# Attention scores in bursts of three doubles, as 64-row matmuls in two halves of the array, over six PSUM banks

## What is computed

```python
scores = (1 / S) * np.matmul(z, z.transpose(0, 2, 1))      # z: (8, 3072, 64)
attn = np.maximum(scores, 0.0) ** 2
x = (u * np.matmul(attn, v)).reshape(B * S, D)             # u, v: (8, 3072, 256)

expert_idx = np.argmax(x @ w_gate, axis=1)                 # 8 experts
for i in range(N):                                         # rows in order, up to capacity each
    if counts[e] < capacity: disp[e, counts[e]] = x[i]; ...
h = np.maximum(np.einsum('ecd,edf->ecf', disp, w1), 0.0)   # w1: (8, 256, 1024)
y = np.einsum('ecf,efd->ecd', h, w2)
out[i] = gate_w[i] * y[expert_idx[i], pos[i]]              # rows that were kept, the rest 0
```

## Time and profile before

| | |
|---|---|
| median of three runs | 867.1 us |
| span of the profiled execution | 865.3 us |
| TensorE matmul busy | 853.5 us |
| TensorE weight load busy | 683.9 us |
| VectorE busy | 632.4 us |
| ScalarE busy | 574.7 us |
| GpSimd busy | 123.2 us |
| attention, until about | 609 us |

### The profile page before, as it was taken

How to read it: one execution, slowest core, us unless ns; L and a number is a source line. 1 busy time by engine, 2 the same in 40 slices (tenths; PEclk the granted TensorE clock), 3 DMA queues, 4 the chain that set the end, 5 groups by cost and what they waited for, 6 DMA issues and landing times.

```text
span 865.3 us, 22736 instructions
## 1 busy us (share of the span) xinstructions
PE 853.5 (99%) x7258; PEld 683.9 (79%) x7259; DVE 632.4 (73%) x1380; ACT 574.7 (66%) x874; POOL 123.2 (14%) x121
## 2 busy tenths in 40 slices
PE   6999999999999999999999999999999999999997
PEld 5888888888888888888888888888777777777776
DVE  7976777988889878887888798687464655565531
ACT  7978786868778779777778777678434434435422
POOL 1001102101101110110110110110112121211212
PEclk9999999999999999999999999999999999999999
DMA  7922343343312633312313313731625325415101
GB/s 274 372 70 94 87 129 136 100 135 117 118 46 97 240 108 97 115 49 92 115 50 98 107 53 108 264 82 40 145 65 171 102 80 158 142 46 152 55 18 36
DMA packets 104277, 98.62 MB, mean 114 GB/s; under 512 B 67149, under 2 KB 91802, under 8 KB 103232
## 3 DMA queue, kind: packets, MB, share of 16 engines
q1 hardware_dynamic: 99360, 85.71, 32.1%
q0 software_dynamic: 4896, 12.64, 4.0%
HBM read 40.03 MB, written 44.93 MB: 98 GB/s over the span
## 4 chain that ended last, share of the span: by engine, by line
PE 97%; DVE 2%; issue 1%; POOL 0%; ACT 0%; POOLq 0%; DVEq 0%; ACTq 0%
PE O L676 17%; PE O L678 17%; PE O L680 17%; PE Sc L786 14%; PE Sc L640 8%; PE Sc L641 8%; PE O L809 3%; PE O L813 3%; PE O L811 3%; PE M L809 2%; PE M L813 2%; PE M L811 2%; PE M L717 1%; PE M L615 0%; DVE zQ L904 0%
## 5 line engine op out<-in xcount | busy, mean ns | idle before, releaser
L676 PE MATMUL O<-vS,attn_hi 128*128 128x256 f16 x1332 | 363.0, 273 | 0.3 <-DVE vS L930 0.3
L680 PE MATMUL O<-vS,attn_lo 128*128 128x256 f16 x1332 | 363.0, 273 | 0.0
L678 PE MATMUL O<-vS,attn_hi 128*128 128x256 f16 x1332 | 363.0, 273 | 0.0
L462 ACT ACTIVATE Sc<-Sc 128x768 f32<-128x768 f32 x224 | 178.0, 795 | 86.3 <-PE Sc L641 78.4
L947 DVE TENSOR_TENSOR attn_lo<-attn,attn_hi 128x768 f16<-128x768 f32 x223 | 213.7, 958 | 7.7
L466 ACT ACTIVATE attn<-Sc 128x768 f32<-128x768 f32 x224 | 181.7, 811 | 7.1
L676 PEld LDWEIGHTS O<-vS,attn_hi 128*128 128x128 f16 x1332 | 130.2, 98 | 27.2 <-issue 0.4
L678 PEld LDWEIGHTS O<-vS,attn_hi 128*128 128x128 f16 x1332 | 130.3, 98 | 26.6
L640 PE MATMUL Sc<-zP 128*128 (+1 forms) x450 | 146.4, 326 | 2.1 <-DVE zP L911 1.3
L641 PE MATMUL Sc<-zQ,zP 128*128 (+1 forms) x450 | 146.4, 326 | 0.0
L941 DVE CAST attn_hi<-attn 128x768 f16<-128x768 f32 x223 | 123.7, 555 | 27.4 <-ACT attn L466 26.0
(11 more groups left out here) (155 smaller groups left out, 912.4 us busy)
## 6 DMA issues: line engine op xcount, KB each, us to landing
out<-empty SPq DMA_DIRECT2D x16, 1536.0 KB, 6.3
wraw<-in_moe_w SPq DMA_DIRECT2D x16, 1024.0 KB, 7.0
rawv<-in_v SPq DMA_DIRECT2D x14, 768.0 KB, 8.5
ubuf<-in_u SPq DMA_DIRECT2D x19, 384.0 KB, 3.1
disp<-vS SPq DMA_DIRECT2D x8, 774.0 KB, 9.1
rawz<-in_z SPq DMA_DIRECT2D x3, 768.0 KB, 6.0
xT<-xrow SPq DMA_TRANSPOSE x54, 2.4
disp<-xrow,slot POOLq DMA_INDIRECT x54, 2.8
```

Source lines behind the costliest of these rows:

```text
L462: act.activation(pair, pair, ACT.Relu).then_inc(s["relu_done"], 1)
L676: nc.tensor.matmul(o_part(t), hi, v[:, 0:D], start=c == 0 and j == 0 and t % 2 == 0, stop=False, skip_group_check=True)
L678: nc.tensor.matmul(o_part(t), hi, v[:, D:2 * D], start=False, stop=False, skip_group_check=True)
L680: ins = nc.tensor.matmul(o_part(t), lo, v[:, 0:D], start=False, stop=c == PAIRS - 1 and j == 1, skip_group_check=True)
```

## The change

Scores are computed as 64-row matmuls. For each double, each of its two key tiles has one half of the array (rows 0 to 63 for the first, 64 to 127 for the second) and a bank of its own, and gets three terms: high keys x high queries, high x low, low x high. The term low x low is gone. Each term is issued for both halves in turn. Three doubles are issued in one burst, at c = 0, 3, 6 and 9 (double c + 3 and the two after it), into six banks, so that PSUM has no banks left for `M`: logits, counts and norm sums lie in the first score bank, and the waits for that are new. Value matmuls keep their 128 rows.

Relu writes from PSUM to `attn`, square works there in place; the score banks wait for relu only. ScalarE's and VectorE's programs are reordered to the bursts, and VectorE's cast waits for the values of four doubles back (`weighed`). The queries of a group are copied by SyncE's DMAs into fixed buffers (`q_now` for the group, `q_next` and `k_next` for the first burst of the next one, which is issued at the end of the group before). The end of the loop is tested after double 6 instead of 5. `identh` is gone; `before` serves in its place. Some small tiles share memory now.

```diff
-LEAD = 3
+BURST = 3
+COUNTS_FROM = 48
+RING = 4
...
-        zsq = sb("zsq", [P, S // 2], BF16)
+        q_now = [sb(f"q_now{k}", [P, GROUP], F16) for k in range(2)]
+        q_next = [sb(f"q_next{k}", [P, GROUP], F16) for k in range(2)]
+        k_next = [sb(f"k_next{k}", [P, SLICE * P], F16) for k in range(2)]
...
-        identh = sb("identh", [P, P], F16)
...
-        Sp = ps("Sc", [P, 4, 512], F32)
-        Mp = ps("M", [P, 2, 512], F32)
+        Sp = ps("Sc", [P, 2 * BURST, 512], F32)
+
+        def half(r):
+            return slice(64 * r, 64 * r + 64)
+
+        def score_banks(c):
+            return slice(2 * (c % BURST), 2 * (c % BURST) + 2)
...
+        small_logits = Sp[:, 0, 0:TILES * 2 * E]
+        small_counts = Sp[:, 0, COUNTS_FROM:COUNTS_FROM + (TILES + 1) * E]
+        norm_sums = Sp[:, 0, 0:GROUP]
...
+            def queries(to, m, loaded):
+
+                for q, z16 in zip(to, (zP, zQ)):
+                    sp.dma_start(q[:, :], z16[:, bass.ds((m & 15) * GROUP, GROUP)]).then_inc(s[loaded], 16)
+
+            def first_keys(m):
+
+                for k, z16 in zip(k_next, (zP, zQ)):
+                    sp.dma_start(k[:, :], z16[:, bass.ds((m & 8) * (S // 8), SLICE * P)]
+                                 ).then_inc(s["loaded_k_next"], 16)
+
             def body(n, end):
                 g = n & 7
-                if not isinstance(n, int):
-
+                if isinstance(n, int):
+                    for key in ("khi_ready", "klo_ready"):
+                        sp.wait_ge(s[key], 2)
+                    first_keys(0)
+                else:
+
+                    wait_apart(sp, s["scores_ready"], n * PAIRS)
+                    queries(q_now, n, "loaded_q_now")
+                    wait_apart(sp, s["scores_ready"], n * PAIRS + BURST)
+                    for key in ("khi_ready", "klo_ready"):
+                        wait_apart(sp, s[key], ((n + 1) & 126) + 2)
+                    queries(q_next, n + 1, "loaded_q_next")
+                    only_if(sp, g == 7, lambda: first_keys(n + 1))
                     for t in range(TILES):
...
             def do_relu(K, c):
                 act.wait_ge(s["scores_ready"], K + 1)
-                pair = Sp[:, 2 * (c % 2):2 * (c % 2) + 2, 0:GROUP]
-                act.activation(pair, pair, ACT.Relu).then_inc(s["relu_done"], 1)
+                if not isinstance(K, int) or K >= BUFS:
+                    wait_apart(act, s["lo_done"], K - BUFS + 1)
+                act.activation(attn[:, c % BUFS, :, :], Sp[:, score_banks(c), 0:GROUP], ACT.Relu
+                               ).then_inc(s["relu_done"], 1)
 
             def do_square(K, c):
                 act.wait_ge(s["relu_done"], K + 1)
-                act.activation(attn[:, c % BUFS, :, :], Sp[:, 2 * (c % 2):2 * (c % 2) + 2, 0:GROUP], ACT.Square,
-                               scale=ROOT_C).then_inc(s["square_done"], 1)
+                act.activation(attn[:, c % BUFS, :, :], attn[:, c % BUFS, :, :], ACT.Square, scale=ROOT_C
+                               ).then_inc(s["square_done"], 1)
...
+                        if not peeled and c == L1_AT:
+                            for t in range(TILES):
+                                act.wait_ge(s["evac_done"], n * 2 - 1 + t // 2)
+                                act.activation(halves[:, t, D:2 * D], ubuf[:, t, :], ACT.Abs, accum_out=l1[:, t:t + 1]
+                                               ).then_inc(s["l1_ready"], 1)
+                        if peeled:
+                            do_relu(K0 + c + 2, c + 2)
+                            do_square(K0 + c + 2, c + 2)
+                            if c == PAIRS - 1:
+                                do_relu(K0 + c + 3, c + 3)
+                                do_square(K0 + c + 3, c + 3)
+                        elif c % BURST == 0:
+                            do_relu(K0 + c + 3, c + 3)
+                        elif c % BURST == 1:
+                            do_relu(K0 + c + 3, c + 3)
+                            do_relu(K0 + c + 4, c + 4)
+                        if not peeled and c == ROWS_HI_AT:
+                            act.wait_ge(s["rscale_ready"], n)
+                            for t in range(TILES):
+                                act.activation(halves[:, t, 0:D], ubuf[:, t, :], ACT.Copy, scale=rscale[:, t:t + 1]
+                                               ).then_inc(s["rows_hi"], 1)
+                        if not peeled:
+                            do_square(K0 + c + 3, c + 3)
...
             def scores(K, n, c, par):
 
 
-                if not (isinstance(K, int) and K < 2):
-                    if par is None:
-                        wait_apart(pe, s["square_done"], K - 1)
-                    else:
-                        pe.wait_ge(s["square_done"], K - 1)
-                qb = (n & 15) * GROUP
-                for j in range(2):
-                    at = (2 * c + j) * P
-                    kb = (n & 8) * (S // 8) + at if par is None else par * S + at
-                    keys, to = zP[:, bass.ds(kb, P)], Sp[:, 2 * (c % 2) + j, 0:GROUP]
-                    nc.tensor.matmul(to, keys, zP[:, bass.ds(qb, GROUP)], start=True, stop=False)
-                    ins = nc.tensor.matmul(to, keys, zQ[:, bass.ds(qb, GROUP)], start=False, stop=True)
+                if not isinstance(K, int):
+                    wait_apart(pe, s["relu_done"], K - BURST + 1)
+                elif K >= BURST:
+                    pe.wait_ge(s["relu_done"], K - BURST + 1)
+
+                def key_cols(z16, k_first, r):
+                    at = (2 * c + r) * P
+                    return k_first[half(r), at:at + P] if par is None else z16[half(r), par * S + at:par * S + at + P]
+
+                def query_cols(z16, q_first, q_rest, r):
+                    if isinstance(n, int):
+                        return z16[half(r), n * GROUP:(n + 1) * GROUP]
+                    return (q_first if par is None else q_rest)[half(r), :]
+
+                high_keys, low_keys = (
+                    [key_cols((zP, zQ)[x], k_next[x], r) for x, r in ((h, 0), (1 - h, 1))] for h in range(2))
+                high_queries, low_queries = (
+                    [query_cols((zP, zQ)[x], q_next[x], q_now[x], r) for x, r in ((h, 0), (1 - h, 1))] for h in range(2))
+                terms = ((high_keys, high_queries), (high_keys, low_queries), (low_keys, high_queries))
+                for at, (keys, queries) in enumerate(terms):
+                    for r in range(2):
+                        ins = nc.tensor.matmul(Sp[:, 2 * (c % BURST) + r, 0:GROUP], keys[r], queries[r],
+                                               start=at == 0, stop=at == len(terms) - 1)
                 ins.then_inc(s["scores_ready"], 1)
...
+            for c in range(BURST):
+                scores(c, 0, c, 0)
+            turn_over(90)
...
+                        def burst():
+                            first = c + BURST
+                            if first < PAIRS:
+                                if peeled:
+                                    wait_keys(2 * (first // BURST) + 2, False)
+                                elif first == PAIRS - BURST:
+                                    wait_keys((n & 120) + 8)
+                                for k in range(first, first + BURST):
+                                    scores(K0 + k, n, k, par)
+                            else:
                                 if not peeled:
                                     wait_keys(((n + 1) & 120) + 6)
-                            scores(K0 + c + LEAD, n + 1, c + LEAD - PAIRS, 0 if peeled else None)
+                                for k in range(BURST):
+                                    scores(K0 + PAIRS + k, n + 1, k, 0 if peeled else None)
+
+                        if not peeled and c == 0:
+                            wait_apart(pe, s["loaded_q_now"], n * 32)
+                        if not peeled and c == PAIRS - 2 * BURST:
+                            wait_apart(pe, s["counts_read"], n)
+                        if not peeled and c == PAIRS - BURST:
+                            wait_apart(pe, s["loaded_q_next"], n * 32)
+                            wait_apart(pe, s["loaded_k_next"], ((n + 1) & 120) * 4 + 32)
+                            only_if(pe, g == 3, lambda: wait_apart(pe, s["nrm_done"], (n & 120) + 8))
+                        if c % BURST == 0 and not (peeled and c == 0):
+                            burst()
...
+                            if c % BURST != BURST - 1 and t == TILES - 1:
+                                ins.then_inc(s["weighed"], 1)
                             if not peeled and (c, t) == LOGITS_AT:
+                                wait_apart(pe, s["relu_done"], K0 + 2 * BURST + 1)
...
+                                wait_apart(pe, s["relu_done"], K0 + 3 * BURST + 1)
+                                norms(zsq).then_inc(s["nrm_psum"], 8)
...
+            def do_hi(K, c, n=0):
                 b = c % BUFS
```

(33 more changed lines are left out.)

93 lines of the change are left out of this document (33 added, 60 removed).

## The result

The changed kernel takes 873.7 us (median of 4 runs, 872.5 to 874.8) against 867.1 us before (4 runs beside it, 867.06 to 867.18): a ratio of 1.0075, 95% interval 1.0061 to 1.0089. It is slower, by 6.6 us; the forecast was 853.9 us. The span of the profiled execution is 871.4 us, its mean granted clock 0.997.

What follows compares the result with a forecast made beforehand. TensorE bounds, busy 853.5 of 865.3 us. Terms -35.3 + 1.97 + 13.7 + 1.7 + 4 + 1 - 0.25 = -13.2 give a span of 852.1 and a median of 853.9 us; range 836 to 874.

Steps and rivals of the forecast that it cites:

- Order inside a group: Layout of a group's steps: all hidden but the counts read before double 6's burst, 0.1 us for 17 groups, +1.7 us.
- rival (c): Burst of double 6: a new wait for the counts takes the gain, 0.7 us in 17 groups; 864 us, chance 0.09.
- Loads: SyncE's query copies: hidden in usual groups, late in the two that load the next batch; +4 us, 1 to 7.
- Norms: Norm sums wait in score bank 0 in two groups: +1 us.
- Scores and switches: Score matmuls: -35.3 us from 64-row halves, +13.7 us for 152 switches between 64-row and 128-row matmuls.
- Both halves at once: Score matmuls: the two 64-row halves run together, so a double takes 0.487 us instead of 0.65.
- The switch: Between 64-row and 128-row matmuls: 0.09 us each, 152 times, +13.7 us; bounds 0 and +39.8.
- (a): Every switch between 64-row and 128-row matmuls empties the pipeline and reloads, 0.262 us: 880 us; chance 0.14.
- (b): Score halves run serially, 965 us, or their weight loads are exposed, 870 to 921 us; chance 0.08.
- (d): Score bursts: the switch is nearly free and weight loads are hidden, 837 us; chance 0.14.
- The three waits: TensorE's waits for the counts read, query copies and norm sums: +1.7, +4 and +1 us.
- slower: Sign of the whole change: slower than before, chance 0.21, against faster 0.74 and same 0.05.

Runs made afterwards that it cites:

- c7: c6 with the counts read put back behind VectorE's exponential sums, as in the changed kernel: 861.96 us, ratio 0.9943.
- c6: c4 plus group 0's last key splits one double later and first expert rows fetched before the wait for the next queries: 852.19 us, ratio 0.9827.
- e1: Changed kernel with VectorE's two steps that read the counts moved ahead of the exponential sums: 870.84 us, ratio 1.0038.
- e5: Changed kernel with the counts read put between the second and third of the four exponential-sum steps: 871.3 us, single run.
- x1: Changed kernel with each double's scores as four 128-row matmuls, its bursts, banks, copies and waits kept: 889.85 us, ratio 1.0269.
- y1: c6 with each double's scores as four 128-row matmuls instead of six 64-row ones: 872.35 us, ratio 1.0059.
- c4: Changed kernel with counts read first, next group's query copies ahead of SyncE's other waits, and norm sums read one double earlier: 858.83 us, ratio 0.9905.
- x4: Changed kernel with one double's scores at a time instead of bursts of three, 24 switches a group instead of 8: 918.08 us, ratio 1.0591.
- x2: Changed kernel with each double's three terms for rows 0-63 issued first, then those for rows 64-127: 876.57 us, single run.

## Why the prediction was wrong

**The step that failed is "Order inside a group", its last paragraph.** The layout was good: TensorE was to be ready for the burst of double 6 at T+15.50 and the counts read at T+15.4. If T is taken from the logits (251.86 = T+11.16), TensorE was ready at T+15.5, its burst was due at T+15.6, and the read was at T+15.4. But I took a semaphore that comes at the due time as free, and put 0.1 us for it. It costs 0.57: behind the wait for the counts TensorE's sequencer has two register steps and three more waits to pass, and the first matmul stands about 0.79 us behind the read; only a read that much ahead of the due time (here by T+14.8) is hidden. Seventeen groups, and 9.8 us instead of 1.7 (c7 against c6).

That the read's place decides is shown by e1, e5 and c7; that the steps behind the wait make up the 0.79 us is read from the trace, and the run that would test it, the wait for the counts put behind the other three, was not made.

The outcome was my rival (c), with 12 us as the bound and a chance of 0.09; what I held against it, that switches relax it, is what x1 refutes.

No row of the trace of before could tell the price: TensorE waited there only in group 0, by waits that stand right before their matmul. One of them, with ScalarE's square ending at 16.91:

```profile
16.96 0.34 PE L640 MATMUL Sc<-zP 128*128 128x384 f16 x1 [0.78 <-ACT attn L466]
```

There it lost 0.05 us, at the others 0.15 us at most. In the loop no wait of TensorE shows as late.

**Loads.** The place and the cause were forecast (groups 9 and 17, behind v and the fill), with +4 in a range of 1 to 7 us. What came is 8.8 us, from the periods over 31.25: 4.3 in group 9, 3.3 in group 17 and 1.2 in group 2, where I had said hidden. (Groups 10 and 16 are 0.2 us longer too, but they are so in c6, where the copies are early.) Two things were missing: the 1.2 GHz level after a stall (1.2 us on the burst of group 9 and some tenths behind it), and group 2.

**Norms.** +1 forecast, 0.62 + 1.46 = 2.1 us over what the norm matmuls take anyway (the gaps before the last bursts of groups 3 and 11); 0.7 of it stays in c6. It is the same loss again: the burst of group 11 starts 0.79 us behind the end of the norm read (VectorE, L1254), with three more waits between.

**Scores and switches.** Both halves at once: right. The switch, 0.09 us: 0.20 - 0.11 before a burst and 1.57 - 1.46 behind it, 0.1 each. For equal counts the forecast is 228 x (0.4875 - 0.65) + 13.7 = -23.4 us, c6 against y1 gives -20.2. So 3 us of the miss are in the switches and the steps, which together gave 0.27 a burst instead of 0.31. Rivals (a), (b) and (d) are out. The Trainium skill, TensorEngine Tiling (Array Packing), section Tiling Modes (Key Properties), says that changing the tiling mode drains TensorE. I had weighed that with a range up to 0.262 us a switch; the runs show 0.1.
The Trainium skill, TensorE: Matmul & The Clock Gate, section Part 3 (The mechanism), says that a weight load overlaps running matmuls only where the row groups differ. Again this isn't seen: y1's full-row bursts keep 12 matmuls in 1.95 us, 0.1625 each, with no place for the load's 0.098.

**More work at the end.** The three more doubles of scores (+1.95) and one of values (+1.97) are 3.9 of the 5.2 us that y1 has over the kernel before; the rest is about 0.5 of the norm wait and 0.8 us that I had not: between the last attention matmul and the expert stage a small matmul (L707, L711 in c4 and c6) starts 0.79 us late, in the new order alone. By the waits view above it waits for ScalarE's end of its loop (L613): the last steps of ScalarE's program come later in the new order.

**Group 0** gained nothing: 0.9 us for a relu behind key splits, of which I had said nothing.

The terms as the runs show them: -20.2 (scores and switches), +1.95, +1.97, +9.8 (counts), +8.8 (copies), +2.1 (norms), +0.9 (group 0), +0.8 (the step before the experts): +6.1 us. The spans of the two profiled executions differ by 871.4 - 865.3 = 6.1, the medians by 6.6. The three waits were sized with 6.7 us instead of 20.7, which is 14 of the 19.8 us between forecast and result; 3.2 lie in scores and switches. That the forecast of 853.9 us comes near c6's 852.2 is luck: without its 6.7 us of waits the forecast would be 847.2, 5 us less than the change gives with the waits taken away. The time lay in the range, 836 to 874, the sign was the other one; the probability for "slower" (0.21) was laid on (a) and (b), while waits of modest size sufficed together.

## What to carry to other kernels

When an edit puts a semaphore in front of the engine that bounds, count its slack to the time at which the wait has to pass for the steps behind it to be done in time, not to that at which the instruction would start: here 0.79 us earlier, for two register steps and three waits. A wait that may come late is best the last before its matmul (not tested here, but the waits of group 0 lost 0.05 us). Look for such a wait under "issue" with nothing late beside it, and take it away by reading the shared buffer before work that nobody waits for. And remove all waits of a loop together before judging one: one can cover the next, as e1 with 2.9 us and c7 with 9.8 us for the same edit show.

## What the runs showed of the hardware

- A late semaphore costs by what stands between its wait and the matmul in TensorE's program. With two register steps and three met waits between, the matmul started 0.79 to 0.83 us after the end of the VectorE instruction that set it (c7 253.95 to 254.75; changed kernel 256.07 to 256.86); with one register step and one wait, 0.38 us after the landing of a DMA (305.58 to 305.96); with nothing between, 0.05 us after the end of a ScalarE instruction (28.99 to 29.05). With the semaphore earlier, nothing is seen of it (c6: gap 0.21).
- A switch between 64-row and 128-row matmuls costs 0.1 us in either direction, at 8 (changed kernel) and at 24 a group (x4).
- Two 64-row halves run at once even if their matmuls are issued one half after the other: 1.58 us a burst in x2, 1.57 in the changed kernel.
- After a stall of 2.64 us TensorE was granted 0.52 of its clock (the 1.2 GHz level) from 306.1 to 309.4. After one of 3.2 us in group 17 it was granted 1.00, while in e1 the stalls of both groups were followed by 0.50; why they differ stays open.
